# Moving the first chunk's operand splits behind the last attention head in a fused attention and feed-forward kernel

## The chip, the cores and the metric

The kernel runs on one core of one Trainium2 chip. The metric is the device time of one execution in microseconds (us); less is better. The median of several executions is compared.

## What is computed

```python
def reference(**kwargs):
    attn_out = _attn_ref(**attn_kwargs)        # 4 batches, 8 heads, 576 positions, 64 wide
    x = attn_out.transpose(0, 2, 1, 3).reshape(2304, 512)
    x = _moe_ref(x=x, **moe_kwargs)            # (gelu(x @ w_in)) @ w_out, 512 -> 2048 -> 512
    return _moe2_ref(x=x, **moe2_kwargs)       # the same shapes, g = clipped square of h

# attention: scores = q k^T / 8 - slope[h] * |i - j|, for 0 <= i - j < 128, softmax, times v
# _moe2: g = h where h >= 1, 0 where h <= -1, (h + 1)^2 / 4 between
```

All of it is in 32-bit floats. The 4 x 8 heads are treated as 16 pairs of heads.

## The kernel before

TensorE is called PE here. The kernel gives it its operands as fp32r, a rounded form. So each operand is held as two parts: `hi`, the rounded number, and `lo`, the number minus `hi`. A product is made of three matrix multiplications, hi*hi, hi*lo and lo*hi (in the scores, hi and lo of the queries lie in the two halves of the partitions). Making `lo` is called a *split* here; it is one subtraction of two tensors in SBUF.

**Attention.** The 16 pairs `q` run as 80 steps `m`, five for each pair (`ORDER`, L49): steps of block kind `d` = 2, 3, 0, 1, 4 (`STEP_ORDER`), kind 0 being the tail rows of both heads. Of each step PE makes the scores (`scores`, L963), DVE adds the bias and takes the maximum (`bias_scores`, L1544; instruction lines L1556 for the tail and L1562), ACT takes the exponential (`exponentials`, L1201; L1207 for the tail, L1212), PE transposes the probabilities (L1001), ACT copies them back (`copy_transposed`, L1237), and PE weighs the values (`weigh_values`, L1004). DVE divides by the sums and writes the pair (`write_pair`, L1567, five steps after the pair's last), PE transposes it (L1031, L1036), ACT and DVE copy it (L1235, L1583), and SP stores it in DRAM as `xd`.

**The operands of the scores.** For every head DVE rounds keys and queries (`round_head`, L1533, the CAST of L1538), and then POOL, the GpSimd engine, splits them: the keys (L885) and, from head 4 on, the queries (L889). PE waits for a head's splits before step d = 2 (first head of the pair) and d = 3 (second head).

**Two feed-forward layers.** They are cut into `PHASES` = 4, each with 3 chunks of 768 tokens up (512 to a part of 2048) and 3 down. Each chunk is a 2 x 2 block product made of 7 block products instead of 8 (`P1` to `P7`). They need 7 operands of the chunk, A11, S1, S2, A12, S3, S4 and A22, of which the S are sums and differences of quadrants, and 7 of each weight pair `w`, built in `w_first` and `w_rest` from the staged `wst`. Each operand is summed (by `sum_operand`, on POOL by `sum_s3` and `sum_s4`), rounded on ACT (`round_operand`, L1271, instruction L1278; `round_weights`, L1242: part 0 is the first of seven, L1262, part 1 the other six, L1265), and split (DVE L1672 and `split_weights`, POOL L911 and L927). PE's order within a product group (a *duo*, `D`) is in `duo`, L1139. Accumulators of later products are *seeded* with copies of earlier ones by ACT (`seed_b`, L1303, `seed_c`, `copy_d`).

**How the two meet.** While the attention runs, POOL also prepares the first chunk and the first weights. What it does is written out by head in its main loop (L934 to L949), always behind the two splits of that head, and each engine executes its list in order. The semaphores `w_added`, `w_rounded`, `w_ready`, `sums_made`, `hi_made` and `lo_made` count up along one fixed order of weights (`MADE`) and operands. DVE does its share at fixed steps `m` (L1656 to L1662), ACT as well (L1294 to L1301). PE takes the first product P1 of the first chunk into the end of the attention (steps 80 and 81, `first_product_1`), then `duo` 0, in which the last pair's transposes (`transpose_pair`, `transpose_pair_tail`) stand between products.

Of the kernel before, what the change touches and what calls it, by code (L numbers as in the profile page):

```python
# [22 lines left out]
ALU = mybir.AluOpType  # L23
# [90 lines left out]
def build(nc, qkT, v_main, v_tail, w_pairs, bias_table, identity, out):  # L114
# [300 lines left out]
    def nth(w):  # L415

        return MADE.index(w)
# [23 lines left out]
    def made_first(w):  # L441
        if w not in STOCK:
            return w_place(w)[:, 0]
        if in_up(w) is None:
            at = g[:, 0, 0, 0:4 * P]
        else:
            at = raw_first[:, 2, 2 * HALF:2 * HALF + 4 * P]
        return at.rearrange("p (h n) -> p h n", h=2).bitcast(F32R)
# [16 lines left out]
    def w_b11(w):  # L465
        return wst[:, 11 if odd(w) else 0]

    def w_others(w):
        return wst[:, 4:10] if odd(w) else wst[:, 2:8]
# [398 lines left out]
    def _(pool):  # L868
# [32 lines left out]
            nc.gpsimd.tensor_tensor(to, a, b, ALU.subtract).then_inc(w_added, 1)  # L901
            pool.wait_ge(w_added, 3 * nth(w) + step + 1)

        def split_weights(w, step):
            pool.wait_ge(w_rounded, 2 * nth(w) + (1 if step == 0 else 2))
            if step == 0:
                to, a, hi = made_first(w)[:, 1], w_b11(w), made_first(w)[:, 0]
            else:
                some = slice(3 * step - 3, 3 * step)
                to, a, hi = made_rest(w)[:, some, 1], w_others(w)[:, some], made_rest(w)[:, some, 0]  # L910
            nc.gpsimd.tensor_tensor(to, a, f32(hi), ALU.subtract).then_inc(w_ready, 1)  # L911
            pool.wait_ge(w_ready, 3 * nth(w) + step + 1)

        def sum_s3():
            pool.wait_ge(sums_made, 2)
# [18 lines left out]
        for head in range(2, 2 * PAIR_COUNT):  # L934
            split_head(head)
            if head == 11:
                add_weights(0, 0)
            if head == 13:
                add_weights(0, 1)
                add_weights(0, 2)  # L940
            if head in (15, 17, 19):
                split_weights(0, (15, 17, 19).index(head))
            if head == 23:
                split_weights(1, 0)
            if head == 25:
                add_weights(1, 1)
                add_weights(1, 2)
            if head in (21, 27, 29, 31):
                split_operand((A11, S1, S2, A12)[(21, 27, 29, 31).index(head)])  # L949
        sum_s3()  # L950
        sum_s4()
        split_operand(S3)
        split_operand(S4)
# [3 lines left out]
    def _(pe):  # L957
# [105 lines left out]
        def weights_ready(w):  # L1063
            if w in STOCK:
                pe.wait_ge(w_loaded[w % W_SLOTS], 16 * OPS * sum(v % W_SLOTS == w % W_SLOTS and v <= w for v in STOCK))
            else:
                pe.wait_ge(w_ready, 3 * (nth(w) + 1))

        def product_1(u, up, c, k, D, n):
            pos = positions(D)[n]  # L1070
            pe.wait_ge(lo_made, OPS * k + A11 + 1)
            if D == 1:

                pe.wait_ge(pair_tail_copied, PAIR_COUNT)
            if up and c == 0:
                weights_ready(8 * u + 2 * (D % DUOS % 2) + pos)
            if not up and c == 0 and n == 0:
                for w in range(8 * u + PAIRS, 8 * u + 2 * PAIRS):
                    weights_ready(w)
            wait_past(pe, c21_out, 2 * (D - 1) + n)  # L1080
            multiply(u, up, k, D, P1, pos, a_bank(D, pos), True).then_inc(p1_done, 1)

        def product_5(u, up, c, k, D, n):
            pos = positions(D)[n]
            pe.wait_ge(lo_made, OPS * k + S1 + 1)
            wait_past(pe, d_copied, 2 * D + n)
            multiply(u, up, k, D, P5, pos, d_bank(D, pos), True).then_inc(p5_done, 1)

        def product_6(u, up, c, k, D, n):
            pos = positions(D)[n]  # L1090
            pe.wait_ge(lo_made, OPS * k + S2 + 1)
            pe.wait_ge(seeded_b, 2 * D + n + 1)
            last = multiply(u, up, k, D, P6, pos, a_bank(D, pos), False)
            if n:
                last.then_inc(p6_done, 1)
# [101 lines left out]
    def _(act):  # L1197
# [86 lines left out]
        for m in range(ALL_STEPS + TRANSPOSE_LAG):  # L1284
            for gi, (_, last_step) in enumerate(GROUPS):
                if last_step == m - TRANSPOSE_LAG:
                    copy_transposed(gi)
            if m < ALL_STEPS:
                exponentials(m)
            if m in (3, 6, 11):  # L1290
                make_bias((3, 6, 11).index(m) + 1)
            if (q := pair_at(m, COPY_LAG)) is not None:
                copy_pair(q)
            if m in (30, 46):  # L1294
                round_weights((30, 46).index(m), 0)
            if m in (32, 72):
                round_weights((32, 72).index(m), 1)
            if m in (44, 64, 69, 74, 77, 79):
                round_operand(0, (44, 64, 69, 74, 77, 79).index(m))
            if m == ALL_STEPS:  # L1300
                round_both(2)  # L1301

        def seed_b(D, n):  # L1303

# [87 lines left out]
        def up(u, c):  # L1392
# [6 lines left out]
                round_weights(w + 2, 0)  # L1399
            copy_d(D, 0)  # L1400
            if D == 0:
                copy_pair(PAIR_COUNT - 1)
            if k:
                round_operand(k, S3)
# [100 lines left out]
    def _(dve):  # L1505
# [140 lines left out]
        for m in range(ALL_STEPS + COPY_TAIL_LAG - 1):  # L1646
# [6 lines left out]
                split_rest()  # L1653
            if m in (1, 2):
                round_head(m + 1)
            if m == 47:  # L1656
                add_first_weights(1)
            if m in (62, 67):
                sum_operand(0, S1 if m == 62 else S2)
            if m == ALL_STEPS:  # L1660
                split_other_weights(1)
                add_weights(2)  # L1662
# [304 lines left out]
```

## Time and profile before

| | us |
|---|---|
| median of 3 executions | 868.41 |
| lowest and highest | 866.93, 868.88 |
| time of the profiled execution | 868.52 |
| its span, first to last instruction | 866.8 |
| PE busy | 852.4 |
| DVE, ACT, POOL busy | 709.3, 536.2, 122.0 |

The profile page cuts the span into 40 slices: POOL is busy in the first seven (70% and more in all but the first) and has nothing to do after that. PE is at 80% or more throughout. The attention ends and the first duo begins at about 144 us. A busy PE is modelled from the starts of its matrix multiplications, so it is not PE at its peak.

### The profile page before, as it was taken

What the parts mean: (1) busy time and instruction counts of PE and PEld (TensorE: products, weight loads), DVE (VectorE), ACT (ScalarE), POOL (GpSimd) and SP (SyncE); (2) the same over time, 40 slices, a digit from 0 to 9 for tenths busy, and PEclk for the clock granted to TensorE, in tenths of its full rate; (3) what the DMA queues carried; (4) which work ended last, traced back from release to release, by engine and by line L of the source; (5) the groups of instructions that cost most, each with busy time, mean ns of one, the idle gap of its engine ahead of it and who ended that gap; (6) DMA issues with size and microseconds to landing.
All of it is one profiled execution on the core that took longest, in us unless ns stands there. A gap on an engine that the chain in (4) does not pass through costs nothing.

```text
span 866.8 us, 15513 instructions
## 1 busy us (share of the span) xinstructions
PE 852.4 (98%) x5746; PEld 846.2 (98%) x5746; DVE 709.3 (82%) x982; ACT 536.2 (62%) x788; POOL 122.0 (14%) x83
## 2 busy tenths in 40 slices
PE   8999998999999999999999999999999999999998
PEld 7999988999999999999999999999999999999998
DVE  7879895577798868677997988898989788889784
ACT  5887778576775546666844556767556567665441
POOL 4799987000000000000000000000000000000000
PEclk9999999999999999999999999999999999999999
DMA  8988661568567266587775764488556643888812
GB/s 196 216 205 218 178 194 53 221 236 302 192 228 258 98 255 219 209 300 248 262 255 206 266 223 155 146 306 277 206 184 231 228 158 139 290 290 301 308 73 74
DMA packets 63241, 186.45 MB, mean 215 GB/s; under 512 B 7488, under 2 KB 14336, under 8 KB 59328
## 3 DMA queue, kind: packets, MB, share of 16 engines
q1 hardware_dynamic: 63168, 185.46, 63.0%
q8 instruction: 47, 0.77, 0.4%
q14 instruction: 26, 0.21, 0.1%
HBM read 113.09 MB, written 72.35 MB: 214 GB/s over the span
## 4 chain that ended last, share of the span: by engine, by line
PE 89%; POOL 5%; DVE 2%; issue 2%; SPq 1%; ACT 1%; DMA 0%; ACTq 0%; DVEq 0%; POOLq 0%
PE ps L1054 80%; PE ps L1022 3%; PE ps L988 2%; POOL k_lo L885 2%; POOL qk_hi L889 2%; PE ps L1001 2%; POOL arena L927 1%; PE ps L1016 1%; DVE qk_hi L1538 1%; DVE probs L1562 1%; DMA qk_raw<-qkT 0%; PE ps L1031 0%; DVE wst L1601 0%; SPq L574 0%; SPq L573 0%
## 5 line engine op out<-in xcount | busy, mean ns | idle before, releaser
L1054 PE MATMUL ps<-arena,w_first 128*128 128x384 f32 x1764 | 333.2, 338 | 0.9 <-ACT ps L1310 0.8
L1054 PEld LDWEIGHTS ps<-arena,w_first 128*128 128x128 f32 x1764 | 312.2, 189 | 2.3 <-issue 1.7
L1054 PE MATMUL ps<-arena,w_rest 128*128 128x384 f32 x1260 | 240.9, 337 | 0.9 <-ACT ps L1310 0.8
L1054 PEld LDWEIGHTS ps<-arena,w_rest 128*128 128x128 f32 x1260 | 220.2, 188 | 2.0 <-issue 1.8
L1672 DVE TENSOR_TENSOR arena<-raw_first,arena 128x768 fp32r<-128x768 f32 (+1 forms) x114 | 148.9, 1319 | 78.3 <-ACT arena L1278 78.3
L1278 ACT ACTIVATE arena<-raw_first 128x768 fp32r<-128x768 f32 (+1 forms) x120 | 132.0, 1117 | 45.6 <-DVE raw_first L1631 38.8
L1054 PE MATMUL ps<-w_rest,arena 128*128 128x256 f32 x945 | 132.5, 281 | 0.0
L1054 PEld LDWEIGHTS ps<-w_rest,arena 128*128 128x128 f32 x945 | 121.2, 189 | 0.1
L1054 PE MATMUL ps<-w_first,arena 128*128 128x256 f32 x567 | 88.1, 282 | 0.0
L1672 DVE TENSOR_TENSOR arena<-raw_rest,arena 128x1536 fp32r<-128x1536 f32 (+1 forms) x48 | 71.4, 1487 | 11.8 <-ACT arena L1278 11.6
L1054 PEld LDWEIGHTS ps<-w_first,arena 128*128 128x128 f32 x567 | 76.0, 189 | 0.0
L1278 ACT ACTIVATE arena<-raw_rest 128x1536 fp32r<-128x1536 f32 (+1 forms) x48 | 60.9, 1269 | 23.0 <-PE ps L1054 21.0
L1319 ACT ACTIVATE d1s<-ps 128x384 f32<-128x384 f32 (+2 forms) x72 | 35.2, 490 | 42.1 <-PE ps L1054 42.0
L1212 ACT ACTIVATE probs<-probs,neg_max 128x256 f32<-128x256 f32 (+1 forms) x128 | 54.0, 472 | 9.5 <-DVE neg_max L1562 9.5
L1022 PE MATMUL ps<-v_sb,probs_t 128*128 128x65 f32 x448 | 57.3, 268 | 2.5 <-ACT probs_t L1240 1.7
L1562 DVE CUSTOM_DVE_ANT_0 probs<-ps,bias_sb 128x256 f32<-128x256 f32 (+1 forms) x128 | 44.8, 387 | 17.8 <-PE ps L988 13.2
L1022 PEld LDWEIGHTS ps<-v_sb,probs_t 128*128 128x128 f32 x448 | 55.3, 192 | 3.2 <-ACT probs_t L1240 2.0
L988 PE MATMUL ps<-qk_hi 128*128 128x256 f32 x160 | 49.3, 330 | 4.8 <-POOL qk_hi L889 2.8
L1310 ACT ACTIVATE ps<-ps 128x384 f32<-128x384 f32 (+2 forms) x72 | 34.0, 475 | 27.9 <-PE ps L1054 27.9
L1601 DVE TENSOR_TENSOR wst<-wst 128x256 f32<-128x256 f32 (+1 forms) x90 | 47.5, 528 | 2.9
L1240 ACT ACTIVATE probs_t<-ps 128x512 f32<-128x512 f32 x64 | 37.7, 590 | 19.5 <-PE ps L1001 19.4
L885 POOL TENSOR_TENSOR k_lo<-qk_raw,qk_hi 128x576 fp32r<-128x576 f32 x30 | 46.3, 1543 | 12.5 <-DVE qk_hi L1538 10.8
(117 smaller groups left out, 974.1 us busy)
## 6 DMA issues: line engine op xcount, KB each, us to landing
gd<-g SPq DMA_DIRECT2D x24, 1536.0 KB, 6.1
raw_rest<-gd SPq DMA_DIRECT2D x32, 768.0 KB, 5.5
wst<-w_pairs SPq DMA_DIRECT2D x32, 512.0 KB, 6.2
raw_first<-gd SPq DMA_DIRECT2D x16, 768.0 KB, 5.8
yd<-ust SPq DMA_DIRECT2D x6, 1536.0 KB, 6.3
qk_raw<-qkT SPq DMA_DIRECT2D x30, 288.0 KB, 3.9
wd<-ust SPq DMA_DIRECT2D x4, 1536.0 KB, 9.7
raw_first<-yd SPq DMA_DIRECT2D x4, 1536.0 KB, 7.9
```

The lines of the kernel that those rows point to most:

```text
L885: nc.gpsimd.tensor_tensor(k_lo[:, slot], keys(qk_raw, head), f32(keys(qk_hi, head)), ALU.subtract).then_inc(qk_split[slot], 1)
L988: last = nc.tensor.matmul(place, queries, k[:, key0:key0 + BAND], start=n_pass == 0 and (d > 0 or i == 0), stop=n_pass == 1 and (d > 0 or ...
L1022: last = nc.tensor.matmul(o_slot(2 * blk + e), probs_t[:, gi % 2, col:col + P], v_sb[:, h + e, max(blk - 1, 0) + piece], start=piece == 0, ...
L1054: last = nc.tensor.matmul(to, stationary, moving, start=start and n == 0, stop=n == len(steps) - 1, skip_group_check=True)
L1212: last = nc.scalar.activation(at, at, ACT.Exp, bias=neg_max[:, col:col + 1], scale=-1.0)
L1240: nc.scalar.activation(probs_t[:, gi % 2], pt_bank[gi % 2], ACT.Copy).then_inc(pt_copied[gi % 2], 1)
L1278: nc.scalar.activation(operand(k, i)[:, 0], source(k, i), ACT.Copy).then_inc(hi_made, 1)
L1310: nc.scalar.activation(b_bank(D, pos), a_bank(D, pos), ACT.Copy).then_inc(seeded_b, 1)
L1319: nc.scalar.activation(d1(D, pos), d_bank(D, pos), ACT.Copy).then_inc(d_copied, 1)
L1562: last = nc.vector.tensor_tensor_reduce(out=to[:, 0:width], in0=bank[:, i * BAND:i * BAND + width], in1=bias_sb[:, h + e, BAND - width:BAN ...
L1601: nc.vector.tensor_tensor(to, a, b, ALU.subtract).then_inc(w_added, 1)
L1672: nc.vector.tensor_tensor(at[:, 1], source(k, i), f32(at[:, 0]), ALU.subtract).then_inc(lo_made, 1)
```

## The change

POOL's list: the splits of A11, S1, S2 and A12 leave the loop over heads (they stood behind heads 21, 27, 29 and 31) and stand behind the last head, each in its place among the sums S3 and S4. The six larger parts of weight pair 0 are split in four pieces of 3 x 128 columns behind heads 17, 19, 21 and 23, instead of two of 3 x 256 behind 17 and 19. The first part of weight pair 1 is split behind head 25 instead of 23, and its two small subtractions stand behind heads 27 and 29 instead of both behind 25.

The other engines follow: DVE's first subtraction for weight pair 1 moves from step 47 to 57, its sums S1 and S2 from steps 62 and 67 to 72 and 78. ACT rounds S1 at step 74, S2 at 79, A12 and S3 at 80 and S4 within the first duo, ahead of the copy of the last pair; the larger part of weight pair 1 at step 75 instead of 72; and the larger part of weight pair 2 behind the last copy of probabilities instead of ahead of it. PE's P1 of a phase's first chunk waits for the first part of the weights alone, and P5 and P6 for all of them.

```diff
--- before.py
+++ after.py
@@ -901,15 +901,22 @@
             nc.gpsimd.tensor_tensor(to, a, b, ALU.subtract).then_inc(w_added, 1)
             pool.wait_ge(w_added, 3 * nth(w) + step + 1)
 
-        def split_weights(w, step):
-            pool.wait_ge(w_rounded, 2 * nth(w) + (1 if step == 0 else 2))
-            if step == 0:
-                to, a, hi = made_first(w)[:, 1], w_b11(w), made_first(w)[:, 0]
-            else:
-                some = slice(3 * step - 3, 3 * step)
-                to, a, hi = made_rest(w)[:, some, 1], w_others(w)[:, some], made_rest(w)[:, some, 0]
-            nc.gpsimd.tensor_tensor(to, a, f32(hi), ALU.subtract).then_inc(w_ready, 1)
-            pool.wait_ge(w_ready, 3 * nth(w) + step + 1)
+        def split_first(w):
+            pool.wait_ge(w_rounded, 2 * nth(w) + 1)
+            nc.gpsimd.tensor_tensor(made_first(w)[:, 1], w_b11(w), f32(made_first(w)[:, 0]),
+                                    ALU.subtract).then_inc(w_ready, 1)
+            pool.wait_ge(w_ready, 3 * nth(w) + 1)
+
+        def split_others(w, part):
+
+            if part == 0:
+                pool.wait_ge(w_rounded, 2 * nth(w) + 2)
+            some, cols = slice(3 * (part // 2), 3 * (part // 2) + 3), slice(P * (part % 2), P * (part % 2) + P)
+            last = nc.gpsimd.tensor_tensor(made_rest(w)[:, some, 1, cols], w_others(w)[:, some, cols],
+                                           f32(made_rest(w)[:, some, 0, cols]), ALU.subtract)
+            if part % 2:
+                last.then_inc(w_ready, 1)
+                pool.wait_ge(w_ready, 3 * nth(w) + 2 + part // 2)
 
         def sum_s3():
             pool.wait_ge(sums_made, 2)
@@ -938,16 +945,19 @@
             if head == 13:
                 add_weights(0, 1)
                 add_weights(0, 2)
-            if head in (15, 17, 19):
-                split_weights(0, (15, 17, 19).index(head))
-            if head == 23:
-                split_weights(1, 0)
+            if head == 15:
+                split_first(0)
+            if head in (17, 19, 21, 23):
+                split_others(0, (17, 19, 21, 23).index(head))
             if head == 25:
-                add_weights(1, 1)
-                add_weights(1, 2)
-            if head in (21, 27, 29, 31):
-                split_operand((A11, S1, S2, A12)[(21, 27, 29, 31).index(head)])
+                split_first(1)
+            if head in (27, 29):
+                add_weights(1, (27, 29).index(head) + 1)
+        split_operand(A11)
+        split_operand(S1)
         sum_s3()
+        split_operand(S2)
+        split_operand(A12)
         sum_s4()
         split_operand(S3)
         split_operand(S4)
@@ -1066,6 +1076,10 @@
             else:
                 pe.wait_ge(w_ready, 3 * (nth(w) + 1))
 
+        def first_weights_ready(w):
+
+            pe.wait_ge(w_ready, 3 * nth(w) + 1)
+
         def product_1(u, up, c, k, D, n):
             pos = positions(D)[n]
             pe.wait_ge(lo_made, OPS * k + A11 + 1)
@@ -1073,7 +1087,7 @@
 
                 pe.wait_ge(pair_tail_copied, PAIR_COUNT)
             if up and c == 0:
-                weights_ready(8 * u + 2 * (D % DUOS % 2) + pos)
+                first_weights_ready(8 * u + 2 * (D % DUOS % 2) + pos)
             if not up and c == 0 and n == 0:
                 for w in range(8 * u + PAIRS, 8 * u + 2 * PAIRS):
                     weights_ready(w)
@@ -1083,6 +1097,8 @@
         def product_5(u, up, c, k, D, n):
             pos = positions(D)[n]
             pe.wait_ge(lo_made, OPS * k + S1 + 1)
+            if up and c == 0:
+                weights_ready(8 * u + 2 * (D % DUOS % 2) + pos)
             wait_past(pe, d_copied, 2 * D + n)
             multiply(u, up, k, D, P5, pos, d_bank(D, pos), True).then_inc(p5_done, 1)
 
@@ -1090,6 +1106,8 @@
             pos = positions(D)[n]
             pe.wait_ge(lo_made, OPS * k + S2 + 1)
             pe.wait_ge(seeded_b, 2 * D + n + 1)
+            if up and c == 0:
+                weights_ready(8 * u + 2 * (D % DUOS % 2) + pos)
             last = multiply(u, up, k, D, P6, pos, a_bank(D, pos), False)
             if n:
                 last.then_inc(p6_done, 1)
@@ -1293,12 +1311,14 @@
                 copy_pair(q)
             if m in (30, 46):
                 round_weights((30, 46).index(m), 0)
-            if m in (32, 72):
-                round_weights((32, 72).index(m), 1)
-            if m in (44, 64, 69, 74, 77, 79):
-                round_operand(0, (44, 64, 69, 74, 77, 79).index(m))
+            if m in (32, 75):
+                round_weights((32, 75).index(m), 1)
+            if m in (44, 74, 79, ALL_STEPS):
+                round_operand(0, (44, 74, 79, ALL_STEPS).index(m))
             if m == ALL_STEPS:
-                round_both(2)
+                round_weights(2, 0)
+                round_operand(0, S3)
+        round_weights(2, 1)
 
         def seed_b(D, n):
 
@@ -1399,6 +1419,7 @@
                 round_weights(w + 2, 0)
             copy_d(D, 0)
             if D == 0:
+                round_operand(k, S4)
                 copy_pair(PAIR_COUNT - 1)
             if k:
                 round_operand(k, S3)
@@ -1653,10 +1674,10 @@
                 split_rest()
             if m in (1, 2):
                 round_head(m + 1)
-            if m == 47:
+            if m == 57:
                 add_first_weights(1)
-            if m in (62, 67):
-                sum_operand(0, S1 if m == 62 else S2)
+            if m in (72, 78):
+                sum_operand(0, S1 if m == 72 else S2)
             if m == ALL_STEPS:
                 split_other_weights(1)
                 add_weights(2)
```

Two places, in the instructions' own order. POOL at the end of its list, from head 30 on (`k_lo` and `qk_hi` are a head's splits, `arena` an operand of the chunk, `raw_first` a sum), before:

```order
L927 TENSOR_TENSOR arena<-raw_first,arena 128x768
L885 TENSOR_TENSOR k_lo<-qk_raw,qk_hi 128x576
L889 TENSOR_TENSOR qk_hi<-qk_raw,qk_hi 64x576
L885 TENSOR_TENSOR k_lo<-qk_raw,qk_hi 128x576
L889 TENSOR_TENSOR qk_hi<-qk_raw,qk_hi 64x576
L927 TENSOR_TENSOR arena<-raw_first,arena 128x768
L916 TENSOR_TENSOR raw_first<-raw_first 128x2x384
L921 TENSOR_TENSOR raw_first<-raw_first 128x768
L927 TENSOR_TENSOR arena<-raw_first,arena 128x768 x2
```

and with the change:

```order
L901 TENSOR_TENSOR wst<-wst 128x256
L885 TENSOR_TENSOR k_lo<-qk_raw,qk_hi 128x576
L889 TENSOR_TENSOR qk_hi<-qk_raw,qk_hi 64x576
L885 TENSOR_TENSOR k_lo<-qk_raw,qk_hi 128x576
L889 TENSOR_TENSOR qk_hi<-qk_raw,qk_hi 64x576
L934 TENSOR_TENSOR arena<-raw_first,arena 128x768 x2
L923 TENSOR_TENSOR raw_first<-raw_first 128x2x384
L934 TENSOR_TENSOR arena<-raw_first,arena 128x768 x2
L928 TENSOR_TENSOR raw_first<-raw_first 128x768
L934 TENSOR_TENSOR arena<-raw_first,arena 128x768 x2
```

Before, one split stands ahead of head 30 and five operations behind head 31; now a small subtraction stands ahead, and eight operations behind.

ACT at the end of the attention, behind the last exponentials of the attention, step 79 (`arena` is an operand's rounding, `probs_t` a copy of transposed probabilities, `w_first` the weight pair 2, `x_pairs` a pair's copy, `ps` the first seeds), before:

```order
L1278 ACTIVATE arena<-raw_first 128x768
L1240 ACTIVATE probs_t<-ps 128x512
L1262 ACTIVATE w_first<-wst 128x256
L1265 ACTIVATE w_first<-wst 128x6x256
L1240 ACTIVATE probs_t<-ps 128x512
L1235 ACTIVATE x_pairs<-ps 128x512
L1310 ACTIVATE ps<-ps 128x384 x2
L1319 ACTIVATE d1s<-ps 128x384
L1235 ACTIVATE x_pairs<-ps 128x512
```

and with the change:

```order
L1296 ACTIVATE arena<-raw_first 128x768
L1258 ACTIVATE probs_t<-ps 128x512
L1296 ACTIVATE arena<-raw_first 128x768
L1280 ACTIVATE w_first<-wst 128x256
L1296 ACTIVATE arena<-raw_first 128x768
L1258 ACTIVATE probs_t<-ps 128x512
L1253 ACTIVATE x_pairs<-ps 128x512
L1283 ACTIVATE w_first<-wst 128x6x256
L1330 ACTIVATE ps<-ps 128x384 x2
L1339 ACTIVATE d1s<-ps 128x384
L1296 ACTIVATE arena<-raw_first 128x768
L1253 ACTIVATE x_pairs<-ps 128x512
```

The six larger parts of the weight pair (the `128x6x256` row) stood ahead of the last `probs_t` copy and now stand behind it, right ahead of the seeds. Four operand roundings lie in this stretch now, where one did.

## Rows read from the trace of the kernel before

**Rows 1.** Busy time by stretch: us, busy us and instructions of each engine, clock, DMA.
```profile
20.00:40.00 20.00, 20.00 (x182) 19.96 (x182) 15.91 (x58) 16.55 (x41) 16.44 (x12) 1.00 0.96 226
80.00:100.00 20.00, 19.03 (x170) 18.50 (x168) 17.45 (x61) 15.16 (x36) 19.14 (x12) 1.00 0.64 174
...
152.00:160.00 8.00, 8.00 (x40) 7.62 (x39) 5.54 (x12) 2.38 (x5) 0.00 (x0) 0.81 0.19 74
```

**Rows 2.** Waits of PE, 20 to 144 us: total us, times, longest us.
```profile
PE ps L988 <- POOL qk_hi L889: 2.8, 6, 0.7
```

**Rows 3.** ACT's timeline, tail exponentials of pairs 6, 8, 11, 12 and 15.
```profile
62.25 0.45 ACT L1207 ACTIVATE probs_tail<-probs_tail,neg_max 128x192 f32<-128x192 f32 x1
...
78.89 0.45 ACT L1207 ACTIVATE probs_tail<-probs_tail,neg_max 128x192 f32<-128x192 f32 x1
...
104.86 0.45 ACT L1207 ACTIVATE probs_tail<-probs_tail,neg_max 128x192 f32<-128x192 f32 x1
...
112.93 0.45 ACT L1207 ACTIVATE probs_tail<-probs_tail,neg_max 128x192 f32<-128x192 f32 x1
...
140.28 0.45 ACT L1207 ACTIVATE probs_tail<-probs_tail,neg_max 128x192 f32<-128x192 f32 x1
```

**Rows 4.** POOL's timeline, one pair (heads 22, 23) and the split ahead of it.
```profile
91.90 2.22 POOL L927 TENSOR_TENSOR arena<-raw_first,arena 128x768 fp32r<-128x768 f32 x1
94.20 1.82 POOL L885 TENSOR_TENSOR k_lo<-qk_raw,qk_hi 128x576 fp32r<-128x576 f32 x1
96.10 1.41 POOL L889 TENSOR_TENSOR qk_hi<-qk_raw,qk_hi 64x576 fp32r<-64x576 f32 x1
97.59 1.43 POOL L885 TENSOR_TENSOR k_lo<-qk_raw,qk_hi 128x576 fp32r<-128x576 f32 x1
99.09 1.40 POOL L889 TENSOR_TENSOR qk_hi<-qk_raw,qk_hi 64x576 fp32r<-64x576 f32 x1
```

**Rows 5.** POOL by form, 20 to 150 us: busy us, mean ns, idle before.
```profile
L927 POOL TENSOR_TENSOR arena<-raw_first,arena 128x768 fp32r<-128x768 f32 x6 | 12.2, 2027 | 3.0 <-ACT arena L1278 2.8
...
L901 POOL TENSOR_TENSOR wst<-wst 128x256 f32<-128x256 f32 x4 | 3.6, 906 | 0.4
```

**Rows 6.** DVE's timeline, two-input operations and casts, alone and beside POOL.
```profile
59.59 0.76 DVE L1538 CAST qk_hi<-qk_raw 128x1152 fp32r<-128x1152 f32 x1
...
74.40 2.00 DVE L1538 CAST qk_hi<-qk_raw 128x1152 fp32r<-128x1152 f32 x1
...
112.44 1.89 DVE L1626 TENSOR_TENSOR raw_first<-raw_first 128x768 f32<-128x768 f32 x1
...
143.48 1.99 DVE L1615 TENSOR_TENSOR w_first<-wst,w_first 128x768 fp32r<-128x768 f32 x2
145.59 3.03 DVE L1601 TENSOR_TENSOR wst<-wst 128x512 f32<-128x512 f32 x3
...
158.16 1.61 DVE L1601 TENSOR_TENSOR wst<-wst 128x512 f32<-128x512 f32 x3
...
175.85 0.96 DVE L1631 TENSOR_TENSOR raw_first<-raw_first,raw_rest 128x768 f32<-128x768 f32 x1
```

**Rows 7.** Timeline of PE and ACT from the last head's scores to the seeds.
```profile
135.97 0.39 PE L988 MATMUL ps<-qk_hi 128*128 128x256 f32 x1 [0.33 <-POOL qk_hi L889]
...
142.53 1.08 PE L1022 MATMUL ps<-v_sb,probs_t 128*128 128x65 f32 x8 [0.23 <-DVE heads_out L1575]
...
148.65 1.48 ACT L1265 ACTIVATE w_first<-wst 128x1536 fp32r<-128x1536 f32 x1 [3.11 <-DVE wst L1601]
...
150.67 1.20 PE L1022 MATMUL ps<-v_sb,probs_t 128*128 128x65 f32 x8 [1.67 <-ACT probs_t L1240]
150.99 0.87 ACT L1310 ACTIVATE ps<-ps 128x384 f32<-128x384 f32 x2
```

**Rows 8.** Chain of work that ended last, 144 to 180 us: start, us, what.
```profile
152.08 3.47 PE ps L1054 x12
...
157.63 22.50 PE ps L1054 x128
```

## The prediction

> **What bounds the kernel now.** I read the busy time by stretch first. PE is busy all of 20 to 40 us with POOL at 16.44 of 20, but between 80 and 100 us POOL is busy 19.14 of 20 and PE falls to 19.03 [rows 1]. PE's busy time is modelled and hides most of a wait: the waits of PE name POOL's query splits with only 2.8 us [rows 2]. So I went by the pace of the pairs. The tail exponential comes once a pair. Between pairs 6 and 8 it takes 78.89 - 62.25 = 16.64 us for two, and the fastest pair, 11 to 12, takes 112.93 - 104.86 = 8.07. From pair 8 to pair 15 it is 140.28 - 78.89 = 61.39 us, or 8.77 a pair [rows 3].
>
> POOL's timeline shows why. The four splits of a pair's two heads run from 94.20 to 100.49 without a gap, 6.29 us, and the operand split ahead of them takes 2.30 with the step between; the next operation starts at 100.58, so this pair costs 8.68 us [rows 4]. PE starts the scores of the last head's step at 135.97, released by POOL [rows 7]. Where POOL's list is under 8.07 us per pair, PE and what feeds it set the pace; where it is over, POOL does. Behind the attention a second loss stands: PE waits 1.67 us at 150.67 for the last copy of probabilities, which ACT had queued behind the rounding of weight pair 2 (148.65, itself 3.11 us late, by DVE) [rows 7]. After it the granted clock is 0.81 for 8 us [rows 1], and 12 multiplications take 3.47 us [rows 8], where at full clock 128 take 22.50, or 2.11 for 12 [rows 8]. From 157.63 PE runs on in one piece; whatever arrives there earlier moves the end by as much.
>
> I measure against the time at which PE starts the last head's scores, T = 135.97; that is 4.31 us ahead of the tail exponential of pair 15.
>
> **Part A, the pairs.** POOL sheds four splits of 2.03 us [rows 5] in the loop, and the waits ahead of three of them (2.8 us in all six [rows 5]). Four pieces of 384 columns take the place of two of 768. No row has such a piece. The mean of 256 columns is 0.906 us and of 768 is 2.027 [rows 5]; on that line 384 is 0.906 + 1.121 / 4 = 1.19 us. The bounds are 0.91 and 1.82, the slower 576 column split [rows 4]. I take 1.19, since it is nearest to the 256. POOL's pair is then 6.29 + 1.19 + gaps of 0.17 = 7.65 us, under 8.07; at 1.82 it is 8.28. The pairs with one subtraction of 256 columns are shorter still (7.4), and the last has nothing behind it. DVE's first subtraction for weight pair 1 is only moved, but it and sum S1 now fall on pairs that are no longer held by POOL. The sum took 1.89 us beside POOL's work against 0.96 for the same width alone [rows 6]; I charge 0.4 for each of the two, half of the shorter one, as DVE still has gaps (17.45 busy of 20 [rows 1]); the bounds are 0 and 1.9. So from pair 8 to 15, four pairs at 8.15 (casts are still stretched now and then: 0.76 us against 2.00 [rows 6]), three at 8.07, and 0.8 make 57.6 us in place of 61.39: a gain of 3.8. The floor is 7 x 8.07 = 56.5, a gain of 4.9. Pair 8 itself is ahead of the first edit that matters.
>
> **Part B, sum S2 at step 78.** It stands ahead of DVE's write of pair 14, and PE already waits 0.23 us for that write at 142.53 [rows 7]. S2 needs the split of S1, which POOL ends at T + 2 x (2.03 + 0.08) = T + 4.2, ahead of DVE's step 78 at about T + 5. So nothing queues on that wait, but the sum's 0.96 us goes straight on the path: +0.9 (1.9 if it is stretched), and everything of DVE behind it is as much later.
>
> **Part C, the last copy.** ACT no longer holds it, so the 1.67 us go. What is late next is the seed: the rounding of weight pair 2 now stands between the copy and the seeds, and waits for the same three DVE subtractions, which end at 148.62 [rows 6], T + 12.65. They come 0.9 later by part B, and the two splits ahead of them (1.99 us [rows 6]) now run beside POOL's chunk work; the subtractions already did, 3.03 us against 1.61 [rows 6]. I add 0.8: T + 14.35. Rounding 1.5 and the first seed 0.45 give T + 16.3. Behind it stand P6 (6 multiplications, 1.05), pair 15's transposes and marks (0.9), P5 (1.05) and the tail's transpose (0.1): T + 19.4 for the point that is 157.63 = T + 21.66 now, a gain of 2.3 with part B in it. That is at full clock. If PE's shorter waits (here I still count some 2 us in pieces) let the clock fall as now, 3.47 - 2.11 = 1.4 come back. I take half: 1.5, between 0.8 and 2.3.
>
> **Part D, costed at nothing.** POOL's eight operations behind the last head end at about T + 20: A11 and S1 at 4.2; sum S3 waits for DVE's S2 until 6 and ends at 8; S2, whose rounding ACT reaches at about 9.9, at 12; A12 at 14, sum S4 at 16, S3 at 18, S4 at 20. PE wants S1 at 15, S2 at 16.3, A12 at 20.5, S3 at 21.5 and S4 at 24.7. The cover is PE's own attention steps and P1; the thinnest margin is 3.5 us, at S3. S4's rounding stands ahead of ACT's copy of pair 15, and waits for a sum that is 2 us early. Uncovered, each late operation costs its 2.0. P1's weaker wait and P5's full one free nothing: the weight splits are done by then. No DMA is added, and the load of weight pair 2 waits for a split that ends near 100 us, ahead of its turn.
>
> **A rule against the change.** The casts and sums of rows 6 take about twice as long while POOL works: 2.00 against 0.76, 1.89 against 0.96. The Trainium skill says so (GPSIMD Engine Reference, "8. Key points"): GpSimd shares its SBUF interfaces with VectorE and contends with VectorE's instructions that have two SBUF inputs or a 2-port mode. By that rule the change puts POOL's eight operations beside exactly such DVE work at the transition; it is the first rival.
>
> The sum is 3.8 + 1.5 = 5.3: 868.5 of the profiled execution less 5.3 is **863.2**. The median of the runs is 0.1 below that execution, which I leave out.
>
> **The rivals.** (1) *DVE slowed by POOL becomes the bound, slower than before.* The pairs then stay near 8.6 us (a gain of 7 x 0.17 = 1.2). At the transition S2 takes 1.9, the two splits 3.8 and the subtractions 3.03 and more, so they end near T + 17, the point of T + 21.66 comes at T + 22.5, and the clock gives back another 1.4: a loss of 2.3. In all +1.1: 869.6. It decides once the subtractions end later than T + 16.6 by the sum of part C at full clock, plus what the pairs gained. For it: rows 6. Against: POOL is idle in part of T + 8 to T + 10. (2) *The pairs gain only half.* DVE's two operations and stretched casts hold a pair at 8.5: 61.39 - 59.5 = 1.9, and 0.8 behind: 865.8. For it: pairs 7 and 8 took 8.32 on average with little on POOL [rows 3]. (3) *The pieces don't get cheaper.* A strided piece costs like a 576 column split, POOL's pair is 8.28, and 4 x 0.15 more are lost, with some waiting: 864.5. (4) *All goes.* Floor pairs and full clock: 868.5 - 4.9 - 2.3 = 861.3. (5) *No change:* POOL's tail makes S3 or S4 late by 3 us and more and gives back what the pairs gained: 867.9.
>
> **Chances.** Forecast 0.48, (1) 0.06, (2) 0.14, (3) 0.10, (4) 0.14, (5) 0.08. A measurement tells about 0.2% from no change, 1.7 us. Faster by more: the forecast, (3), (4) and most of (2), 0.84. Same: (5) and the rest of (2), 0.10. Slower: 0.06. The range takes in (2) and (4): 861.0 to 866.4.
>
> **What would show it.** Of the profile after: tail exponentials of pairs 8 to 15 some 57.6 us apart in place of 61.4; POOL with idle gaps before each pair's first split; the pieces at 1.2 us; no wait of PE for ACT's copy, but one of up to a microsecond for the write of pair 14 and one for a seed; the point that is 157.63 now at 152.3. The forecast is wrong if the pairs don't speed up, if DVE's subtractions for weight pair 2 end later than T + 16, or if PE waits for POOL's S2, S3 or S4.

## The result and the profile after

The changed kernel takes 865.58 us (median of 7 executions, 864.22 to 865.84) against 868.41 of the kernel before (7, 866.93 to 869.74). The ratio is 0.9966, with a 95% interval of 0.9954 to 0.9977: 2.8 us faster, where 5.3 were forecast. The profiled execution took 865.84 us, its span is 864.1. Executions of either kernel come in two groups by the mean clock granted to PE: two of the seven of the changed kernel kept 1.00 and took 864.22 and 864.48 us, the others had 0.996 to 0.998 and took 865.53 to 865.84, and those of the kernel before lie near 867 and from 868.4 up in the same way, so each median depends a little on how many of its executions lost clock.

**The pairs.** Busy time by stretch, columns as in [rows 1]:

```profile
80.00:100.00 20.00, 20.00 (x183) 20.00 (x182) 18.20 (x62) 16.54 (x38) 17.24 (x13) 1.00 0.69 183
144.00:152.00 8.00, 5.57 (x38) 5.18 (x37) 7.67 (x10) 3.96 (x7) 5.96 (x4) 0.95 0.18 71
152.00:160.00 8.00, 8.00 (x40) 7.55 (x39) 2.51 (x6) 4.48 (x7) 1.56 (x1) 0.84 0.23 60
```

PE is busy all of 80 to 100 us, where it had 19.03, and POOL falls from 19.14 to 17.24. The transition, from the end of the attention into the first products, is no better: between 144 and 152 us PE is busy 5.57 of 8, and behind it the mean granted clock is 0.84 over 8 us, as it was 0.81. The row of 144 to 152 us of the kernel before is

```profile
144.00:152.00 8.00, 6.33 (x47) 5.97 (x46) 4.53 (x6) 4.75 (x9) 2.25 (x1) 0.97 0.35 104
```

ACT's timeline: tail exponentials of pairs 6, 8 and 15, as [rows 3], and the rounding that now stands ahead of the last of them:

```profile
62.46 0.45 ACT L1225 ACTIVATE probs_tail<-probs_tail,neg_max 128x192 f32<-128x192 f32 x1
...
78.74 0.45 ACT L1225 ACTIVATE probs_tail<-probs_tail,neg_max 128x192 f32<-128x192 f32 x1
...
133.87 1.47 ACT L1283 ACTIVATE w_first<-wst 128x1536 fp32r<-128x1536 f32 x1
...
137.47 0.46 ACT L1225 ACTIVATE probs_tail<-probs_tail,neg_max 128x192 f32<-128x192 f32 x1
```

From pair 8 to 15 it is 137.47 - 78.74 = 58.7 us in place of 61.4. But these marks are late at times by what ACT has ahead of them: it rounds weight pair 1 (133.87, 1.47 us) at step 75 now. DVE's bias of the same tail, which ACT waits for, is the cleaner mark. In the timeline of DVE of the kernel before it stands, for pairs 8 and 15, at

```profile
78.49 0.34 DVE L1556 CUSTOM_DVE_ANT_0 probs_tail<-ps,bias_tail 128x192 f32<-128x192 f32 x1
...
138.69 0.36 DVE L1556 CUSTOM_DVE_ANT_0 probs_tail<-ps,bias_tail 128x192 f32<-128x192 f32 x1 [0.98 <-PE ps L988]
```

and in that of the changed kernel at

```profile
77.82 0.34 DVE L1577 CUSTOM_DVE_ANT_0 probs_tail<-ps,bias_tail 128x192 f32<-128x192 f32 x1
...
134.66 0.36 DVE L1577 CUSTOM_DVE_ANT_0 probs_tail<-ps,bias_tail 128x192 f32<-128x192 f32 x1 [0.98 <-PE ps L998]
```

so the last pair is 4.03 us earlier. Of that, 0.67 us are there at pair 8 already, and from pair 8 to 15 it is 56.84 us in place of 60.20, a gain of 3.36. PE starts the last head's scores at T' = 131.96 where T was 135.97:

```profile
131.96 0.36 PE L998 MATMUL ps<-qk_hi 128*128 128x256 f32 x1
```

POOL's timeline for one pair and the piece ahead of it, which answers to [rows 4]:

```profile
90.39 1.01 POOL L915 TENSOR_TENSOR w_first<-wst,w_first 128x384 fp32r<-128x384 f32 x1
92.10 1.43 POOL L885 TENSOR_TENSOR k_lo<-qk_raw,qk_hi 128x576 fp32r<-128x576 f32 x1 [0.70 <-DVE qk_hi L1559]
93.61 1.81 POOL L889 TENSOR_TENSOR qk_hi<-qk_raw,qk_hi 64x576 fp32r<-64x576 f32 x1
95.50 1.42 POOL L885 TENSOR_TENSOR k_lo<-qk_raw,qk_hi 128x576 fp32r<-128x576 f32 x1
96.99 1.41 POOL L889 TENSOR_TENSOR qk_hi<-qk_raw,qk_hi 64x576 fp32r<-64x576 f32 x1
```

The piece takes 1.01 us in place of 2.22, and a gap of 0.70 opens ahead of the next head: POOL waits for DVE now, not PE for POOL.

**The transition.** POOL's timeline behind the last head:

```profile
131.55 3.74 POOL L934 TENSOR_TENSOR arena<-raw_first,arena 128x768 fp32r<-128x768 f32 x2
137.95 1.81 POOL L923 TENSOR_TENSOR raw_first<-raw_first 128x768 f32<-128x768 f32 x1 [2.66 <-DVE raw_first L1652]
141.50 4.33 POOL L934 TENSOR_TENSOR arena<-raw_first,arena 128x768 fp32r<-128x768 f32 x2 [1.74 <-ACT arena L1296]
145.91 1.89 POOL L928 TENSOR_TENSOR raw_first<-raw_first 128x768 f32<-128x768 f32 x1
147.88 1.88 POOL L934 TENSOR_TENSOR arena<-raw_first,arena 128x768 fp32r<-128x768 f32 x1
```

and DVE's beside it (sum S2, the write of pair 14, the two splits of weight pair 1, the three subtractions of weight pair 2):

```profile
136.85 0.95 DVE L1652 TENSOR_TENSOR raw_first<-raw_first 128x768 f32<-128x768 f32 x1
...
138.17 0.82 DVE L1596 TENSOR_TENSOR heads_out<-ps,inverse 128x640 f32<-128x640 f32 x1
...
140.08 1.83 DVE L1636 TENSOR_TENSOR w_first<-wst,w_first 128x768 fp32r<-128x768 f32 x2
142.01 6.08 DVE L1622 TENSOR_TENSOR wst<-wst 128x512 f32<-128x512 f32 x3
```

The three subtractions take 6.08 us; they took 3.03 before and take 1.61 alone [rows 6]. The staging tile's own rows, with the shortest, the median and the longest of them in ns, first before:

```profile
L1601 DVE TENSOR_TENSOR wst<-wst x3: 424/425/2114, 145.6 to 148.2; 128x256 f32<-128x256 f32 x2, 128x512 f32<-128x512 f32 x1
```

and after:

```profile
L1622 DVE TENSOR_TENSOR wst<-wst x3: 1933/1937/2142, 142.0 to 146.2; 128x256 f32<-128x256 f32 x2, 128x512 f32<-128x512 f32 x1
```

Before, one of the three was long, 2.11 us, while POOL worked on one split, and the two of 256 columns took 0.42. After, all three take 1.93 us or more, the 256 column ones about as long as one of POOL's instructions (1.9 to 2.2 us). PE and ACT behind them, as [rows 7]:

```profile
148.12 1.48 ACT L1283 ACTIVATE w_first<-wst 128x1536 fp32r<-128x1536 f32 x1 [3.54 <-DVE wst L1622]
...
149.51 0.85 ACT L1330 ACTIVATE ps<-ps 128x384 f32<-128x384 f32 x2
...
150.09 1.35 PE L1064 MATMUL ps<-arena,w_first 128*128 128x384 f32 x6 [2.43 <-POOL arena L934]
```

The rounding waits 3.54 us for the subtractions, the first seed comes at 149.51, and PE waits 2.43 us. The chain of work that ended last, as [rows 8]:

```profile
147.88 1.89 POOL arena L934
...
150.09 1.35 PE ps L1064 x6
...
153.15 1.76 PE ps L1064 x6
...
155.01 25.13 PE ps L1064 x143
```

The point that was 157.63 is 155.01: 2.62 us earlier, of the 2.7 by which the span is shorter. Counted from T it was 21.66; it is 23.05 from T'. So the pairs gave 4.0 us and the transition took 1.4 back.

### The profile page after: what moved, and what is told of

Read it like the earlier page. It is cut to its first block, busy times and chain, and to the rows that moved or that the text cites. A ratio compares the mean times of both kernels' runs of the same rounds, so it can differ in the third digit from the quotient of the medians.

```text
span 864.1 us, 15512 instructions
## 1 busy us (share of the span) xinstructions
PE 851.0 (98%) x5746; PEld 845.7 (98%) x5746; DVE 710.4 (82%) x982; ACT 536.0 (62%) x788; POOL 120.3 (14%) x85
## 4 chain that ended last, share of the span: by engine, by line
PE 93%; DVE 2%; issue 2%; SPq 1%; ACT 1%; POOL 1%; DMA 0%; DVEq 0%; ACTq 0%; POOLq 0%
PE ps L1064 80%; PE ps L1032 4%; PE ps L998 4%; PE ps L1011 3%; PE ps L1041 1%; PE ps L1026 1%; POOL arena L934 1%; DMA qk_raw<-qkT 0%; DVE probs L1583 0%; DVE wst L1622 0%; SPq L574 0%; SPq L573 0%; DVE qk_hi L1559 0%; POOL raw_first L928 0%; DVE w_first L1629 0%
## 5 line engine op out<-in xcount | busy, mean ns | idle before, releaser
L1622 DVE TENSOR_TENSOR wst<-wst 128x256 f32<-128x256 f32 (+1 forms) x90 | 50.6, 562 | 2.9
```

What stands on the lines that cost most here:

```text
L1622: nc.vector.tensor_tensor(to, a, b, ALU.subtract).then_inc(w_added, 1)
```

## The experiments

Each was timed in 5 or more executions beside the kernel before on the same chip. The kernel before had medians of 868.3 (e1 to e4), 867.2 (e5 to e8) and 867.8 us (e9b, e10b), so differences under some 0.5 us between groups are read from the traces rather than from the medians. The lower medians have more executions at a clock of 0.999 or more: 13 of 21 beside e5 to e8, and 4 of 15 beside e1 to e4.

**e3: one part of the change alone.** In the kernel before:

```diff
             if m == ALL_STEPS:
-                round_both(2)
+                round_weights(2, 0)
+        round_weights(2, 1)
```

> The kernel before, with one part of the change alone: ACT rounds the six larger parts of weight pair 2 behind the last copy of probabilities. Theory (what bounds the transition is the time at which ACT reaches the first seed, and PE's waits there bring the lower clock with them): DVE's subtractions still end near 148.6 us, the rounding at 150.1, the first seed at 150.6, P6 can start at 150.7 in place of about 153.8, and the point that is 157.63 comes at 153.8 at full clock, 155.5 at the lower one: 864.6 to 866.4 us. Rival (the gain of the whole change comes from the pairs alone, this order is worth nothing, since the seeds wait for the same subtractions): 868.4.

Measured: 864.83 us, ratio 0.9962 (0.9950 to 0.9975). This one moved line gives 3.5 us by the medians, more than the whole change. Part of that is the clock: four of its five executions kept 1.00, and the two of the changed kernel that did so took 864.22 and 864.48 us, less than the 864.76 at best here. Busy time by stretch, and the chain:

```profile
144.00:152.00 8.00, 8.00 (x59) 7.88 (x58) 6.39 (x12) 5.24 (x9) 2.19 (x1) 1.00 0.34 104
152.00:160.00 8.00, 8.00 (x48) 7.65 (x47) 5.05 (x8) 5.48 (x7) 0.00 (x0) 1.00 0.43 144
```

```profile
149.84 2.11 PE ps L1054 x12
...
154.02 16.00 PE ps L1054 x91
```

PE has no wait there and the clock stays at 1.00. The last values no longer wait for the copy and run at full clock themselves, so the 12 multiplications of P5 and P6 start at 149.84 in place of 152.08, 2.24 us earlier, and they take 2.11 us where they took 3.47 [rows 8], 1.36 less by the clock. Together this is the 3.6 us from 157.63 to 154.02. The seeds come at 149.86, only 1.1 us earlier than before [rows 7], while P5 runs, so P6 does not wait for them.

**e4: the same part undone in the changed kernel.**

```diff
                 round_weights(2, 0)
+                round_weights(2, 1)
                 round_operand(0, S3)
-        round_weights(2, 1)
```

> The changed kernel with the rounding of the larger parts of weight pair 2 put back ahead of the last copy of probabilities (and ahead of S3's rounding). Theory: the copy then waits for DVE's subtractions, which end near 148.1 us there, so PE's last values start near 151.1 and the rest takes the 7.0 us that it took before: about 158.1 in place of 155.0, 868.5 us or a little more. Rival (the order is worth nothing): 865.6.

Measured: 869.43 us, ratio 1.0016 (1.0007 to 1.0025), slower than before. The wait of PE at the transition:

```profile
PE ps L1032 <- ACT probs_t L1258: 5.2, 1, 5.2
```

It was 1.67 us before; the subtractions behind which the copy stands take 6.03 us here. With e3 this makes a table: the order of ACT gives 3.5 us on the old lists of POOL and 3.8 on the new ones (865.6 against 869.4), and the new lists, in which the pairs are 4.0 us faster, cost 1.1 us without ACT's order and 0.8 with it. What the pairs gain is lost at the transition, and more. (The 0.8 is a difference of medians again: e3 kept the clock in most executions, the changed kernel in two of seven.)

**e1: POOL out of DVE's way.** In the changed kernel, POOL:

```diff
         sum_s3()
+        pool.wait_ge(w_added, 3 * (nth(2) + 1))
         split_operand(S2)
```

> The changed kernel with one wait more: POOL does not start the split of S2 until DVE's three subtractions for weight pair 2 are done. Theory (a two-input DVE operation beside POOL's waits out POOL's whole instruction, about 2 us for each, whatever its own width): the three subtractions take 1.6 us in place of 6.1 and end near 143.7, the first seed comes at 146.5, PE no longer waits 2.4 us for it, the point at 155.0 comes at 151.3 to 152.5: 862 to 863 us, though POOL ends 2 us later. Rival 1 (the subtractions are long for a reason of their own, not POOL's work): they still take 6.1 us, and POOL's splits come 6 us later still, so PE waits for S2: 867 or more. Rival 2 (it is POOL's list that is the bound, as the chain of work names it, not the seeds): later splits make it slower, 867.6.

Measured: 861.95 us, ratio 0.9928 (0.9915 to 0.9942). DVE's timeline, the three subtractions,

```profile
141.70 1.61 DVE L1623 TENSOR_TENSOR wst<-wst 128x512 f32<-128x512 f32 x3
```

POOL's, the two splits behind its new wait,

```profile
143.44 3.74 POOL L934 TENSOR_TENSOR arena<-raw_first,arena 128x768 fp32r<-128x768 f32 x2 [3.99 <-DVE wst L1623]
```

and the chain:

```profile
149.88 0.59 ACT x_pairs L1254
...
150.84 19.17 PE ps L1065 x109
```

The subtractions take 1.61 us, as alone. PE's wait for the seed is gone, the clock is 1.00 throughout, and the point is 150.84, T' + 19.2 with T' at 131.66, where part C of the prediction had 19.4. One added wait gives 3.6 us by the medians, some 2.4 of it where the changed kernel kept its clock too (864.22 and 864.48), so POOL's list was not the bound, though the chain of the changed kernel runs over POOL's splits from 141.5 to 149.8.

**e2: the seeds ahead of the rounding.** In the changed kernel, ACT:

```diff
-        round_weights(2, 1)
...
                 copy_pair(PAIR_COUNT - 1)
+                round_weights(2, 1)
```

> The changed kernel with the rounding of the larger parts of weight pair 2 moved further back, behind the seeds and the copy of the last pair. Theory (PE's 2.4 us wait is for the seed, which stands behind this rounding, which waits for DVE): the first seed comes near 145, P6 follows P5 without a wait, and the next thing late is DVE's write of pair 15, which stands behind the subtractions and ends at 149.4 us; the point at 155.0 comes near 152.1: 862.7 us. Rival (the wait is for POOL's split, as the chain of work names it): no change, 865.6.

Measured: 863.14 us, ratio 0.9942 (0.9930 to 0.9955). The subtractions are as long as ever (6.09 us), but only the write of pair 15 waits for them now:

```profile
PE ps L1041 <- DVE x_pairs L1604: 1.2, 1, 1.2
```

The chain reaches the point at 152.22, against 152.1 expected. That the wait was for the seed and not for POOL is shown by this run too, since POOL's operations are where they were.

**e7: as many columns, one instruction more.** In the changed kernel, DVE's `add_weights`:

```diff
                 to, a, b = w_sum(w, step)
+                if w == 2 and step == 0:
+                    nc.vector.tensor_tensor(to[:, 0], a[:, 0], b[:, 0], ALU.subtract)
+                    to, a, b = to[:, 1], a[:, 1], b[:, 1]
```

> The changed kernel with DVE's 512 column subtraction for weight pair 2 cut into two of 256 columns: as many columns, one instruction more. Theory (each two-input DVE instruction waits out one whole POOL instruction): four subtractions take 4 x 1.95 = 7.8 to 8.0 us in place of 6.1, the first seed comes 1.9 us later, PE's wait for it is 4.3 in place of 2.4 us: 867.3 to 868. Rival (POOL and DVE share the columns, and each column costs about twice as much): 6.2 us for the four, 865.7.

Measured: 867.95 us, ratio 1.0004 (0.9995 to 1.0013); the gain of the whole change is gone. DVE's timeline, the four subtractions:

```profile
141.50 1.88 DVE L1623 TENSOR_TENSOR wst<-wst 128x256 f32<-128x256 f32 x1
143.30 5.95 DVE L1625 TENSOR_TENSOR wst<-wst 128x256 f32<-128x256 f32 x3
```

From 141.50 to 149.25 they take 7.75 us, 1.94 each. The price is per instruction and not per column: each ends a little behind the end of one POOL instruction. PE's wait for P6, in the waits of PE:

```profile
PE ps L1064 <- issue: 4.1, 1, 4.1
```

It is 4.1 us, and laid to no engine here, as POOL was idle from 148.96 on.

**e5: the pieces undone.** In the changed kernel, POOL splits three whole parts behind each of heads 17 and 19:

```diff
-            some, cols = slice(3 * (part // 2), 3 * (part // 2) + 3), slice(P * (part % 2), P * (part % 2) + P)
...
+            some = slice(3 * part, 3 * part + 3)
...
-            if head in (17, 19, 21, 23):
-                split_others(0, (17, 19, 21, 23).index(head))
+            if head in (17, 19):
+                split_others(0, (17, 19).index(head))
```

> The changed kernel with one part undone: the six larger parts of weight pair 0 are split in two pieces of 768 columns behind heads 17 and 19, as before, not in four of 384. Theory (a pair holds PE up only where POOL's list for it passes 8.07 us): with 2.03 us for a piece POOL's list is 8.3 to 8.7 us in two pairs, PE starts the last head's scores 0.4 to 1.0 us later than in the changed kernel (at 132.4 to 133.0 in place of 132.0), and the rest shifts with it: 866.0 to 866.6 us. Rival (the four pieces were not needed, the four operand splits were all that held the pairs): 865.6.

Measured: 866.33 us, ratio 0.9987 (0.9978 to 0.9995). The tail bias of pair 15 stands at 135.35 in place of 134.66, and the point at 155.70 in place of 155.01, 0.7 us later in both. PE waits for POOL's splits again:

```profile
PE ps L997 <- POOL qk_hi L889: 0.7, 2, 0.4
```

So the pieces are worth 0.7 us. The other 3.3 of the 4.0 are left for the rest of what changed in the loop, above all the four operand splits taken out of it; no run has these apart.

**e6: sum S2 behind the write of pair 14.** In the kernel of e1, DVE:

```diff
-            if m in (72, 78):
-                sum_operand(0, S1 if m == 72 else S2)
+            if m in (72, 79):
+                sum_operand(0, S1 if m == 72 else S2)
```

> The kernel of e1 (POOL waits for the subtractions), and DVE's sum S2 stands behind the bias of step 79 in place of step 78, so no longer ahead of the write of pair 14. Theory: PE's wait of 0.72 us for that write goes, with nothing in its place: 861.95 - 0.7 = 861.2 us. Rival (it is made up for at the next wait, since the subtractions end as late as before): 861.9.

Measured: 863.75 us, ratio 0.9959 (0.9945 to 0.9972). It is some 1.8 us slower than e1, a miss of both readings. POOL's sum S3 waits for S2 and now falls beside DVE's two splits of weight pair 1:

```profile
140.20 3.27 DVE L1637 TENSOR_TENSOR w_first<-wst,w_first 128x768 fp32r<-128x768 f32 x2
```

They take 3.27 us in place of 1.82, the subtractions end at 145.18 in place of 143.31, POOL starts behind them at 145.31, and its sum S4 ends at 151.05. The copy of pair 15 stands behind S4's rounding on ACT, and PE waits for it:

```profile
PE ps L1047 <- ACT x_pairs L1254: 1.7, 1, 1.7
```

**e8: the copy ahead of S4's rounding, on e6.**

```diff
-                round_operand(k, S4)
                 copy_pair(PAIR_COUNT - 1)
+                round_operand(k, S4)
```

> The kernel of e6, and ACT copies the last pair ahead of S4's rounding instead of behind it. Theory (in e1 the chain runs from POOL's sum S4 at 147.3 over S4's rounding and the copy at 149.9 to PE's tail transpose at 150.5): the copy comes 0.9 us earlier, up to 0.7 us more: 860.5 to 861.0 us. Rival (S4's split is then late for P3, which takes the gain back): 861.2 or more.

Measured: 863.55 us, ratio 0.9955 (0.9943 to 0.9968), no better than e6. The copy's wait is gone and another has come:

```profile
PE ps L1065 <- POOL arena L934: 1.5, 1, 1.5
```

Here the wait is POOL's own. Its last two splits, S3 and S4, run from 151.14 to 156.60, and in the chain the first of them takes 3.22 us, up to 154.36, when P7's products start. (So it is S3's split, not S4's as the expectation of e9b has it.) DVE's split of 1536 columns of weight pair 2, 149.29 to 152.68, lies beside it: the two engines slow each other. Once POOL is put off by another 2 us, its list is the bound.

**e9b: the same, on e1.**

> The kernel of e1 (POOL waits for the subtractions, sum S2 at step 78 again), with ACT's copy of the last pair ahead of S4's rounding. In e1 the products of P5 end at 150.3 us and PE's tail transpose waits 0.2 us for the copy. Theory (e1 has only that wait left, and S4 has slack since its sum ends no earlier than 149.1): 861.95 - 0.3 = 861.7 us, within what can be told from e1. Rival (POOL's list is the next bound, as e8 showed with 1.5 us of wait for S4's split: each delay of S4 costs): 862.0 to 862.6.

Measured: 861.81 us, ratio 0.9932 (0.9919 to 0.9944). PE's only wait of note in the transition is the one for the write of pair 14:

```profile
PE ps L1033 <- DVE heads_out L1597: 0.7, 1, 0.7
```

The point comes at 150.46 in place of 150.84, but by the times it can't be told from e1, as was expected.

**e10b: the changed kernel beside it.** No edit.

> The changed kernel itself, on the chip of e9, so that the two are told apart on one chip: 865.6 us, 3.5 to 4.0 above e9.

Measured: 865.74 us, ratio 0.9981 (0.9966 to 0.9997), 3.9 us above e9b on one chip. Its nine executions spread from 863.91 to 870.00 us, and the two longest, 868.41 and 870.00, have the lowest mean clocks, 0.994 and 0.992.

## Why the prediction was right and where it was off

The measured time lies inside the forecast's range of 861.0 to 866.4 us, near its slow end. The mechanism of the pairs held. That of the transition did not: by the prediction's own sign of being wrong, subtractions that end later than T + 16, it failed, since they ended at T' + 16.1.

**Part A, the pairs: right, and the size in part by luck.** The forecast was 3.8 us at T, measured 4.03; the piece took 1.01 us, where 1.19 was taken. e5 gives the pieces' share, 0.7 us. Three errors made up for each other. ACT's mark of pair 15 was late by 1.2 us in the kernel before (DVE's bias ended at 139.05, the exponential started at 140.28), so the 61.4 us from pair 8 to 15 were 60.20 by DVE's marks. The 0.8 us charged for DVE's moved operations were hardly there: the two intervals of tail marks in which they fall are 8.21 us (102.20 to 110.41) and 8.12 (126.54 to 134.66) against the 8.07 of a fast pair. And pair 8 was not ahead of the first edit that matters: from pair 7 to 8 it takes 8.08 us (69.74 to 77.82) in place of 8.96 (69.53 to 78.49), and 8.96 again in e5 (69.80 to 78.76), where the first piece is as long as before.

**Part B, sum S2: right in kind.** PE waits 0.72 us for the write of pair 14, where it waited 0.23; the forecast was 0.9 more, measured 0.5. e6 shows what the prediction did not see: the place of this sum also sets what POOL's sum S3 collides with.

**Part C, the last copy: the term that was mis-sized.** The wait for the copy went, and the seed was late next, as forecast. But the prediction added 0.8 us for POOL's work beside DVE's and kept the subtractions at 3.03. They took 6.08, so they ended at T' + 16.1 in place of T + 14.35; P6 started at T' + 18.1 in place of 16.3. And half of the clock's loss was taken, where the profiled execution had all of it: from P6 to the point it took 4.9 us, where the sum had 3.1 at full clock and 0.7 for half of the loss. Together 23.05 - 19.4 = 3.65 us against the sum at full clock. Against the forecast, which took a gain of 1.5 us for this part where 1.4 were lost, it is 2.9. Part A gave 0.2 more, so 2.7 were to be missed; the profiled executions miss 2.6 (5.3 forecast, 868.52 - 865.84 = 2.7 measured). e1 takes the first cause away and the second goes with it, as PE no longer stands still for 2.4 us: the point is then at T' + 19.2.

The error was in how the rows were read. The 3.03 us [rows 6] were taken as three operations at twice their time. They were one operation that waited out one POOL instruction and two that met none. With three or four instructions of POOL in line, each DVE operation with two SBUF inputs waits for one. The page's rule (the Trainium skill, GPSIMD Engine Reference, "8. Key points") named the contention rightly, and the trace agrees: 6.08 us beside POOL, 1.61 with POOL standing still. That section gives no size, and by e1 and e7 the size is one POOL instruction for each DVE instruction.

**Part D, costed at nothing: right for this change.** PE waits for none of POOL's operands, by e1 and e2, in which the wait laid to POOL disappears with POOL as late or later. Its margin was thin: in e8, with sum S3 ending 2 us later than in the change and the wait of e1, PE waits 1.5 us for it.

**The rivals.** The first named the mechanism (DVE slowed by POOL, subtractions near T + 17), and that half of it happened; the pairs did not stay slow, so it did not end slower than before. e4 did, at 869.4 us, but by another way: the pairs stay fast, and ACT's old order sets the copy behind the slow subtractions. The second rival has the measured number almost exactly, 865.8 us, and is not what happened: it let the pairs gain 1.9 us and the transition 0.8, where they gained 4.0 and lost 1.4.

## What to carry to other kernels

Where POOL and DVE work side by side on SBUF tensors, count DVE's two-input instructions and not their columns, and keep those that others wait for out of a closed row of POOL instructions: one added wait on POOL was worth 3.6 us here. Try each part of a change alone: here one line of ACT's order was worth more than the whole by the medians, since the other part, a real gain of 4 us on the attention's pairs, moved POOL's work to where it cost more. And the engine that a chain names need not be the one waited for: ask what the waiting instruction reads, and what it adds to. Last, a mark for the pace of a loop should be an operation with nothing else queued ahead of it: ACT's exponential made one stretch 1.2 us too long.

## What the runs showed of the hardware that was not expected

A DVE subtraction of 256 columns took 0.42 us alone and 1.93 beside POOL's back-to-back instructions of 1.9 to 2.2 us, and one of 512 columns 2.14; cutting the latter in two made four instructions of 1.94 us each on average (e7, 7.75 us in all), and letting POOL stand still brought all three back to 1.61 us (e1). It looks as if a DVE instruction that comes while POOL's runs is served only near that one's end; the runs show the times, not the arbiter. It goes the other way as well. POOL's split of 768 columns took 3.22 us (e8) and 3.25 (e1) where DVE's split of 1536 columns ran, and 1.81 to 2.25 in the kernel before; DVE's split took 3.39 us in e8, and 1.75 in the kernel before. The times of e8 look like turns: POOL's sum ends at 151.06, DVE's split 1.6 us later at 152.68, and POOL's split 1.7 us after that at 154.36, each about as long as alone.

The granted clock fell in some of the profiled transitions and not in others. Where it fell it went to 0.50, the level of 1.2 GHz, as between 152 and 154 us in the kernel before and in the change, and it was back at 1.00 from 158 us on. Its mean over 144 to 160 us was 0.89 in the kernel before (longest wait 1.67 us), in both profiles of the changed kernel and in e5 (2.4 to 2.5 us), and 0.79 in e7 and e4 (4.1 and 5.2 us). It stayed at 1.00 in e1, e3 and e9b, with no wait over 0.7 us, in e2 (1.2), and also in e8 (1.5) and e6 (1.7). So the longest wait does not decide alone: 1.67 us cost the clock in the kernel before, and 1.7 did not in e6. No run here tells what does. In the change the fall made 6 multiplications of P5 take 1.76 us, where at full clock 12 take 2.11 (e3); in its second profile (e10b) it fell earlier and those of P6 took 2.26. By the two groups of executions it costs some 1.4 us in the changed kernel, 865.78 in the middle of one group against 864.22 and 864.48.
